# Linear attention, an ELU feed-forward layer and dense experts on one core: weight slices in 16 places of their own, experts in alternate halves, attention inputs three deep, chunk scaling two to three steps earlier

## The reference

```python
# attention, per sequence and head; state is 48 x 48
cur = k_t (outer) v_t
y_t = r_t @ (state + (u * k_t) (outer) v_t)
state = w_t[:, None] * state + cur
# feed-forward, d_ff = 2048, ELU between
h = x @ w_in; g = where(h > 0, h, exp(min(h, 0)) - 1); x = g @ w_out
# four dense experts of 1024, every token through each
p = probs / (probs.sum(-1) + 1e-9)
out += p[:, e] * (relu(x @ w1[e]) @ w2[e])
```

## Time and profile before

| | |
|---|---|
| median of 3 timed runs | 715.22 us (714.51 to 717.27) |
| the profiled execution | 715.24 us, span 713.4 us, mean granted clock 0.978 |
| TensorE matmul busy | 686.0 us, 96% |
| VectorE busy | 268.3 us, 38% |
| ScalarE busy | 179.9 us, 25% |
| GpSimd busy | 140.8 us, 20% |
| first up-projection | 28.62 us |
| DMA | 38.65 MB, mean 54 GB/s |

### The profile page before, as it was taken

One profiled execution on the slowest core, in us unless ns is written; L12 is line 12 of the kernel. 1 busy time (PEld: TensorE's weight loads), 2 busy tenths in 40 slices (PEclk: granted clock), 3 DMA queues, 4 the chain that ended last, 5 costly groups with the idle time before them and its releaser, 6 DMA issues.

```text
span 713.4 us, 10383 instructions
## 1 busy us (share of the span) xinstructions
PE 686.0 (96%) x3964; PEld 610.6 (86%) x3964; DVE 268.3 (38%) x474; ACT 179.9 (25%) x339; POOL 140.8 (20%) x147
## 2 busy tenths in 40 slices
PE   7767999999999999999999999999999999999998
PEld 4667998988888788889999999999999999999997
DVE  7475567766555443331213121221312131212122
ACT  1344443334333544431111111111111111111110
POOL 3242311210110066000003620005600016400000
PEclk9589899999999999999999999999999999999999
DMA  8354342222200023000000310002200002001011
GB/s 306 103 208 145 105 142 80 78 79 78 79 1 1 0 68 103 8 1 1 0 1 23 101 54 1 0 0 67 88 22 0 0 0 88 1 1 44 0 45 45
DMA packets 12851, 38.65 MB, mean 54 GB/s; under 512 B 1552, under 2 KB 3344, under 8 KB 12816
## 3 DMA queue, kind: packets, MB, share of 16 engines
q1 hardware_dynamic: 12528, 37.77, 15.8%
q10 hardware_dynamic: 288, 0.39, 0.2%
HBM read 35.80 MB, written 2.36 MB: 53 GB/s over the span
## 4 chain that ended last, share of the span: by engine, by line
PE 89%; DVE 6%; ACT 2%; DMA 2%; issue 1%; SPq 0%; DVEq 0%
PE bank L828 27%; PE bank L830 26%; PE bank L829 26%; PE bank L789 3%; PE bank L745 2%; PE bank L785 1%; DMA raw<-w_dram 1%; PE bank L756 1%; DVE bank L616 1%; PE bank L769 1%; DVE fr L509 1%; PE bank L800 1%; DVE rkw L532 1%; ACT w_hi L414 1%; DVE rkw L525 1%
## 5 line engine op out<-in xcount | busy, mean ns | idle before, releaser
L828 PE MATMUL bank<-x_lo,w_hi 128*128 128x512 f32 (+2 forms) x480 | 182.5, 380 | 3.8 <-DVE g_lo L622 2.4
L687 DVE SCALAR_TENSOR_TENSOR g_lo<-bank,g_hi 128x512 fp32r<-128x512 f32 x96 | 66.4, 692 | 306.5 <-ACT g_hi L470 306.5
L830 PE MATMUL bank<-x_hi,w_hi 128*128 128x512 f32 (+2 forms) x480 | 179.3, 374 | 0.0
L829 PE MATMUL bank<-x_hi,w_lo 128*128 128x512 f32 (+2 forms) x480 | 179.1, 373 | 0.0
L470 ACT ACTIVATE g_hi<-bank 128x512 fp32r<-128x512 f32 x96 | 57.4, 598 | 339.1 <-PE bank L830 339.1
L830 PE MATMUL bank<-w_hi,g_hi 128*128 128x384 f32 x384 | 129.7, 338 | 0.0
L828 PE MATMUL bank<-w_lo,g_hi 128*128 128x384 f32 x384 | 129.5, 337 | 0.0
L829 PE MATMUL bank<-w_hi,g_lo 128*128 128x384 f32 x384 | 129.4, 337 | 0.0
L828 PEld LDWEIGHTS bank<-x_lo,w_hi 128*128 128x128 f32 x480 | 92.0, 192 | 17.3 <-DVE g_lo L622 3.1
L830 PEld LDWEIGHTS bank<-x_hi,w_hi 128*128 128x128 f32 x480 | 91.9, 191 | 16.1
L829 PEld LDWEIGHTS bank<-x_hi,w_lo 128*128 128x128 f32 x480 | 92.0, 192 | 12.0
(11 more groups left out here) (62 smaller groups left out, 574.4 us busy)
## 6 DMA issues: line engine op xcount, KB each, us to landing
raw<-w_dram SPq DMA_DIRECT2D x48, 384.0 KB, 3.1
rkw<-rkw_dram SPq DMA_DIRECT2D x10, 772.5 KB, 4.5
tok<-tok_dram SPq DMA_DIRECT2D x12, 576.0 KB, 4.7
out_dram<-acc SPq DMA_DIRECT2D x10, 192.0 KB, 1.9
rkw<-rkw_dram SPq DMA_DIRECT2D x2, 512.0 KB, 4.5
rkw<-rkw_dram SPq DMA_DIRECT2D x2, 260.5 KB, 3.7
out_dram<-acc ACTq DMA_DIRECT2D x2, 192.0 KB, 2.2
u_rep<-u_dram SPq DMA_DIRECT2D x1, 192.0 KB, 6.5
```

Of the source, the lines that this page charges most:

```text
L687: dve.scalar_tensor_tensor(out=g2[1][:, r, :], in0=p_h[j % 2][:, :], scalar=0.0, in1=g2[0][:, r, :].bitcast(F32), op0=ALU.max, op1=ALU.sub ...
L828: pe.matmul(out, wh, ml, start=start, stop=False)
L829: pe.matmul(out, wl, mh, start=False, stop=False)
L830: return pe.matmul(out, wh, mh, start=False, stop=stop)
```

## The change

Each of the 16 slots gets its own raw place and semaphore, and the feed-forward slices load without a wait. Expert e uses the slots e % 2 * 8 + j, and its slices load once the slot's last down-projection is done (`load_expert_slice`); GpSimd waits for the landing alone, and the gate product goes. Loops over experts are unrolled. `rkw` and `tok` become three deep (`DEEP`), alpha two deep. Scores of chunk c move to step 4c-1 (7, 11, 15, 19, 23, 27, 31, 35, 39, 43 in place of 5, 10, 15, 20, 24, 28, 32, 36, 40, 44). The scaling of a chunk moves from steps -3, -2, -1, 0 to -5, -4, -3, -2 relative to its scores, behind bonus and scale_state. w_lo of slices 0 and 2 moves from VectorE to GpSimd, which now does every w_lo in two halves. In the prologue TensorE does scores(1), turn_k(1) and update(0) before values(1), and both turn_y last; three of the four bonus products of chunks 0 and 1 go to VectorE, their bonus_v to GpSimd; warm-ups are 5, 1, 1, 1, 1 in place of 5, 2, 1.

```diff
-SCORES = {2: 5, 3: 10, 4: 15, 5: 20, 6: 24, 7: 28, 8: 32, 9: 36, 10: 40, 11: 44}
+SCORES = {c: 4 * c - 1 for c in range(FIRST, NC)}
-LO_VECTOR = (0, 2, 3, 5, 7, 9, 11, 13)
-LO_POOL = (1, 4, 6, 8, 10, 12, 14, 15)
+LO_VECTOR = (3, 5, 7, 9, 11, 13)
+LO_POOL = (0, 1, 2, 4, 6, 8, 10, 12, 14, 15)
-HI_AFTER = {n: n + 5 for n in range(J1 - 5)}
+HI_AFTER = {n: n + 6 for n in range(J1 - 6)}
...
-        raw = sb("raw", [P, STAGE, 2 * DM])
+            raw = sb("raw", [P, J1, 2 * DM], scope=scope)
...
# SyncE
+            def load_expert_slice(e, j):
+                slot = slot_of(e, j)
+                if e < 2:
+                    sp.wait_ge(s_down, STEP1 - J1 + slot + 1 + RING)
+                else:
+                    sp.wait_ge(s_down, STEP1 + (e - 1) * (NT * J2) - J2 + j + 1 + RING)
+                sp.dma_start(raw[:, slot, :], w_d[J1 + e * J2 + j]).then_inc(s_raw[slot], 16)
...
             def load_rkw(c):
-                need(sp, s_py, c - 1)
-                need(sp, s_pkt, c - 1)
+                need(sp, s_py, c - DEEP + 1)
+                need(sp, s_pkt, min(c - DEEP + 1, NUPDATE))
...
-            load_slices(0, 1, 2, 3)
+            load_slices(0, 1, 2, 3, 4, 5)
             load_rkw(2)
-            load_slices(4, 5)
             load_tok(2)
-            load_slices(6, 7, 8)
+            load_slices(6, 7, 8, 9)
             load_rkw(3)
-            load_slices(9)
             load_tok(3)
...
# GpSimd
-                pool.tensor_tensor(w_lo[:, n, :], raw[:, n % STAGE, :], w_hi[:, n, :].bitcast(F32),
-                                   ALU.subtract).then_inc(s_wq, 1)
+                for half in (slice(0, DM), slice(DM, 2 * DM)):
+                    pool.tensor_tensor(w_lo[:, n, half], raw[:, n, half], w_hi[:, n, half].bitcast(F32),
+                                       ALU.subtract).then_inc(s_wq, 1)
...
-            pool.wait_ge(s_u, 16)
-            pool.wait_ge(s_qp, FIRST)
-            bonus_terms(0)
-            bonus_terms(1)
+            landed(pool, s_tok, 0)
+            pool.wait_ge(s_f, FIRST)
+            pool.tensor_tensor(tok[0][:, 0:DM], tok[0][:, 0:DM], tok[0][:, DM:2 * DM], ALU.mult).then_inc(s_rk, 1)
+            pool.wait_ge(s_rk, 2 * FIRST)
+            lo_w(0)
+            bonus_v(0)
+            bonus_v(1)
             lo_w(1)
+            lo_w(2)
             lo_w(4)
             bonus_terms(2)
...
# ScalarE, prologue
             hi_w(2)
+            hi_w(3)
             hi_x(0, BANKS0["yt"])
             hi_x(1, BANKS1["yt"])
-            hi_w(3)
             hi_w(4)
+            hi_w(5)
...
# VectorE, prologue
             scale_r(1)
+            dve.wait_ge(s_u, 16)
+            bonus_product(0, u_rep[:, :], 1)
+            landed(dve, s_tok, 1)
+            bonus_product(1, tok[1][:, DM:2 * DM], 2)
+            bonus_product(1, u_rep[:, :], 3)
             mask_scores(1, BANKS1)
             bonus(0)
-            bonus_v(0)
+            bonus(1)
             finish_y(0, BANKS0)
-            bonus(1)
-            bonus_v(1)
+            finish_y(1, BANKS1)
             lo_x(0, BANKS0["yt"])
-            finish_y(1, BANKS1)
-            lo_w(0)
             lo_x(1, BANKS1["yt"])
-            lo_w(2)
...
# VectorE, steps
-                for c in due(n, 0):
-                    scale_r(c)
                 elu(n)
...
-                for c in due(n, -3):
-                    products(c)
-                for c in due(n, -2):
-                    inverses(c)
-                for c in due(n, -1):
-                    scale_k(c)
                 for c in due(n, 0):
                     bonus(c)
                     scale_state(c)
+                for c in due(n, -5):
+                    products(c)
+                for c in due(n, -4):
+                    inverses(c)
+                for c in due(n, -3):
+                    scale_k(c)
+                for c in due(n, -2):
+                    scale_r(c)
...
# TensorE, prologue
             turn_k(0, BANKS0)
-            warm(2)
+            warm(1, 1)
             values(0, BANKS0)
+            scores(1, BANKS1)
+            turn_k(1, BANKS1)
             update(0, BANKS0)
-            scores(1, BANKS1)
+            warm(1, 2)
+            values(1, BANKS1)
+            update(1, BANKS1)
             turn_y(0, BANKS0)
-            warm(1)
-            values(1, BANKS1)
-            turn_k(1, BANKS1)
+            warm(1, 1)
             turn_y(1, BANKS1)
-            update(1, BANKS1)
+            warm(1, 1)
```

More of the change, by code:

```diff
@@ L56 @@
 NSL = J1 + NE * J2
-STAGE = 4
+DEEP = 3
 RING1 = 3
@@ L109, in bass_linear_attention_elu_ffn_dense_experts @@
             g1 = [sb(f"g1_{i}", [P, RING1, TILE], F32R, scope=scope) for i in ("hi", "lo")]
-            rkw = [sb(f"rkw_{i}", [P, RKW], scope=scope) for i in range(2)]
-            tok = [sb(f"tok{i}", [P, 3 * DM], scope=scope) for i in range(2)]
+            rkw = [sb(f"rkw_{i}", [P, RKW], scope=scope) for i in range(DEEP)]
+            tok = [sb(f"tok{i}", [P, 3 * DM], scope=scope) for i in range(DEEP)]
             u_rep = sb("u_rep", [P, DM], scope=scope)
@@ L371, in _ @@
             lo_w(8)
-            bonus_v(2)
             bonus_terms(3)
             lo_w(10)
+            bonus_v(2)
             lo_w(12)
-            bonus_v(3)
-            bonus_terms(4)
             lo_w(14)
             lo_w(15)
-            bonus_v(4)
-            for c in range(5, NC):
+            bonus_v(3)
+            for c in range(4, NC):
                 bonus_terms(c)
                 bonus_v(c)
-            def expert_slices(e, done):
+            for e in range(NE):
                 for j in range(J2):
[L388 to L396, removed]
+                    split(e, j)
         @block.scalar
@@ L411, in hi_w @@
             def hi_w(n):
-                k = n % STAGE
-                act.wait_ge(s_raw[k], 16 * (n // STAGE + 1))
-                act.copy(w_hi[:, n, :], raw[:, k, :]).then_inc(s_wh, 1)
+                act.wait_ge(s_raw[n], 16)
+                act.copy(w_hi[:, n, :], raw[:, n, :]).then_inc(s_wh, 1)
             copy_kt(0, BANKS0)
@@ L586, in lo_w @@
                 dve.wait_ge(s_wh, n + 1)
-                dve.tensor_tensor(w_lo[:, n, :], raw[:, n % STAGE, :], w_hi[:, n, :].bitcast(F32),
+                dve.tensor_tensor(w_lo[:, n, :], raw[:, n, :], w_hi[:, n, :].bitcast(F32),
                                   ALU.subtract).then_inc(s_wv, 1)
@@ L801, in turn_y, with warm @@
                 ins.then_inc(s_pyt, 1)
-            def warm(times):
+            def warm(times, b):
                 zeros = st[:, :, :, :].rearrange("p c a e -> p (c a e)")
                 for _ in range(times):
-                    pe.matmul(bank[4][:, 0:DM], zeros[:, 0:P], zeros, start=True, stop=True)
+                    pe.matmul(bank[b][:, 0:DM], zeros[:, 0:P], zeros, start=True, stop=True)
             pe.wait_ge(s_zero, 3)
-            warm(WARM_UP)
+            warm(WARM_UP, 1)
             scores(0, BANKS0)
@@ L861, in down2 @@
                     ins = passes(p_acc[b][:, 0:DM], (g2[0][:, r, toks], g2[1][:, r, toks]),
-                                 (w_hi[:, j, DM:2 * DM], w_lo[:, j, DM:2 * DM]), j == 0, j == J2 - 1)
+                                 (w_hi[:, slot, DM:2 * DM], w_lo[:, slot, DM:2 * DM]), j == 0, j == J2 - 1)
                     if j == J2 - 1 and b < TB - 1:
@@ L917, in _ @@
             tile2(0, NT - 1, 0, 1)
-            with pe.Fori(1, NE - 1) as e:
+            for e in range(1, NE):
                 with pe.Fori(0, NT - 1) as T:
                     tile2(e, T, T + 1, e)
-                tile2(e, NT - 1, 0, e + 1)
-            with pe.Fori(0, NT - 1) as T:
-                tile2(NE - 1, T, T + 1, NE - 1)
-            tile2(NE - 1, NT - 1, 0, 0, end=True)
+                tile2(e, NT - 1, 0, e + 1, end=e == NE - 1)
 ORDER = np.concatenate([np.arange(HALF)[::-1], np.arange(HALF, CH)])
```

123 lines of the change are left out of this document (54 added, 69 removed).

## The result

The changed kernel takes 740.78 us (median of 4 runs, 739.37 to 748.88) against 715.88 us (4 runs, 714.51 to 717.27): the ratio is 1.037, 95% interval 1.029 to 1.045. I had forecast 709.7 us, at most 727, and given "slower" 0.28. The raw slices lie in the places of w_lo itself, and the subtraction overwrites them; so a slice may only land once its slot's w_lo is no longer used, and alternate halves leave it the time for that.

What follows compares the result with a forecast made beforehand. TensorE, busy 96% of the span, was taken to bound the kernel. Prologue -7.0, tile 0 -4.0, tile 1 +6.6 and tile 2 -1.1 sum to -5.5: 709.7 us, with an 8 in 10 range of 697 to 727.

Steps and rivals of the forecast that it cites:

- slower: Rival, chance 0.28: holes ahead of values, port 1.7 a chunk, clock falls in two of tile 1's four chunks; 725.9 us.
- Order: VectorE takes inverses(c+1) ahead of the mask that values wait for: 1.4 us idle per chunk in tile 1, without contention.
- Scores' wait: TensorE's scores no longer wait for VectorE's scaled r, 12.4 us in 7 waits before.
- The port: GpSimd and VectorE collide at the moved inverses: only alpha waits, 0.8 us a chunk in tile 1.
- The clock: TensorE's clock falls once, after tile 0's hole at chunk 2, about 2.9 us lost.
- My sum for tile 1: Work of 57.4 plus four values steps of 1.4 + 0.8: 66.4 us against 59.8, +6.6.
- free port: Rival, chance 0.20: no collision of GpSimd and VectorE and no fall of the clock; -15.8, 699.4 us.
- prologue's case: Rival, chance 0.17: clock falls in the prologue anyway, gain 3.5 in place of 7.0; 715.6 us, no change.
- Tile 0: First 16 feed-forward steps, with late masks, port collisions and one clock fall: 62.6 against 66.6 us, -4.0.
- Prologue: Reordered work before the first up-projection, which comes at 21.6 in place of 28.6 us: gain 7.0, otherwise 3.5.
- Loads: Sixteen raw slots and three deep inputs remove SyncE's waits on slices; expert loads stay hidden; costed at nothing.
- Tile 2: Chunk 8's scores leave this tile and the mask comes before TensorE needs it: -1.1 us.

Runs made afterwards that it cites:

- e2: The changed kernel with GpSimd's bonus_v(c) also waiting until VectorE's inverses(c+1) are done, so GpSimd is silent beside them; 724.7 us.
- e4: The changed kernel with 14 extra unused matmuls of 384 columns ahead of values of chunks 2 to 9, filling the hole; 730.4 us.
- e6: The kernel of e1 with the small tile credit four floats wide in place of three, which moves no tile; 706.0 us.
- e7: The kernel of e1 with padding that moves the places of tiles in SBUF, same instructions; 704.3 us.
- e8: The kernel of e6 with the scores' steps of the kernel before; 712.4 us.
- e3: The changed kernel with inverses one step later, at -3 with scale_k, behind the mask of the chunk before; 703.4 us.
- e1: The changed kernel with VectorE's scaling of a chunk back in its old places, all else still changed; 702.6 us.

## Why the prediction was wrong

The place was right and the price was not. By stage the profiled run lies 32.3 us above the forecast: tile 1 by 16.0, tile 0 by 6.3, tile 2 by 5.6, the step time behind step 48 by 2.7, the prologue by 1.8. **Order:** I had values held by mask behind inverses(c+1), 1.4 us of hole in tile 1; e2, without the port, shows 1.5. **Scores' wait:** down from 12.4 to 2.3, as forecast in kind.

**The port, the first step that failed.** I took 0.8 a chunk, "the one that the row does show", and kept 1.7 for the slower case, on the ground that no row showed a scan starting while GpSimd holds. It waits: scan 0.64 and alpha 0.74, 1.4 a chunk, which made the hole 2.9 in place of 2.2; in tile 0 tail waited as well. The rule of the Trainium skill (GPSIMD Engine Reference, section Specifications) pointed there: GpSimd collides with VectorE instructions that have two SBUF inputs or run in a two-port mode. The trace agrees for scan (1.87) and alpha (0.88), which have two; tail (0.90) has one, and whether it runs in such a mode no row shows. Mask, with one operand in PSUM, kept its 1.28.

**The clock, the step that cost most.** The forecast had one fall in all, and the slower rival falls in two of tile 1's four chunks, from holes of "about 3 us". It fell in every chunk of tile 1, and in e2 behind holes of 1.5 us. The price of a fall, 2.9 us, was right (12.2 for four, e4), the count was not: seven falls from tile 0 to tile 2, where the sum has one. With four falls the rival's own sum would have been 57.4 + 12.4 + 11.6 = 81.4 for tile 1, against 82.4 measured. My sum for tile 1 was also added up 0.2 too high: 57.4 and four times 2.2 are 66.2. And the second window of the earlier trace rows does not end at the fall; that came at 70.9, inside the hole. The free port is refuted by the scan's 1.87. The prologue's case is not: the clock fell for 3.4 us in this run, and in e2, e4, e6 and e7 from 13 us up to the first projection, which came at 26.2 to 26.8.

**Tile 0**, forecast at 62.6, took 68.9: its first hole was 5.1 us before values(2) (scan 1.87, alpha 0.88 and tail 0.92 one after another, on top of the late products), and the clock was low from 52.5 to 62.7, longer than the one fall that I paid. A second fall, from 76.4 to 83.2, came behind the hole of 2.9 before values(3).

**Prologue:** 7.0 forecast, 5.2 measured; the bounds 21.6 and 25.1 met 21.2 to 26.8 over the runs with this prologue. Which it is hangs on whether the clock holds near 13 us. **Loads:** nothing, as costed (e8). **Tile 2:** -1.1 forecast, +4.5 measured: the mask came too late there as well (a hole of 1.9 us), and the clock fell once. **Step time:** costed at nothing, it cost 0.046 and 0.02 us a step, 2.7 us behind step 48; e7, with the same loops, shows that the places of the tiles hold most of it.

## What to carry to other kernels

When work is moved earlier on an in-order engine, ask what stood behind the new place and who waits for that: here 1.4 us of scan moved out of the way of scores stood in the way of the mask, and one step further on (e3) it was free. Price a hole in TensorE's stream by what it does to the clock as well as by its length: against e1, tile 1 lost 5.5 us a chunk to holes of 2.9 and 2.8 to holes of 1.5, about twice the hole. When the nearest row shows one op waiting for another engine, give the case in which its neighbours wait too the higher chance. And measure one program twice before a small difference is explained: e1 and e6 are the same and lie 3.3 us apart.

## What the runs showed of the hardware

- VectorE's scan, alpha and scale_k, which have two SBUF inputs, and the small tail copy ran before or after GpSimd's ops here and not beside them; the one that waited goes next, so back-to-back ops of both alternate: alpha's 0.14 became 0.88, GpSimd's 1.0 became 1.92. The reduction (0.54 before, two in 1.00 at 16.5 after) and ops that read PSUM (mask, 1.28) ran on beside GpSimd.
- The granted clock went to 0.50 (1.2 GHz) after each hole of 1.5 us in e2's tile 1 and stayed there for 3.4 us (6.8 the first time); after 2.9 us, for 6.8 each time. With the holes filled (e4) it stayed at 1.00 in tile 1. In e3 it fell twice with no hole before it.
- The places of tiles in SBUF moved a step of 18 matmuls of 512 columns between 4.133 (e7) and 4.193 us (e1) with the same instructions.
- The same prologue code took 21.5 us in e1 and 26.7 and 26.8 in e6 and e7, with the clock at 1.00 in the one and at 0.50 from 13 us on in the others; compare stages, not only totals.
